# Attention, a cos-gated layer and a routed expert layer in one kernel: the loads of queries, keys and values reshaped, and the order of several steps changed

## The reference

```python
for c in range(nc):                                  # chunks of 32 queries
    k_full = concat([mem_k, k[l_start:r_end]]); v_full = concat([mem_v, v[l_start:r_end]])
    a = softmax(scale * q_c @ k_full.T)
    out[c] = a @ v_full
x = out as [3072, 512]
h = x @ w_in                                         # 512 -> 2048
x = (h * cos(h)) @ w_out                             # 2048 -> 512
compute = x @ w_skip > 0
e = argmax(x @ w_gate); g = max(softmax(x @ w_gate))
out = x; out[compute] += g * (relu(x @ w1[e]) @ w2[e])   # 512 -> 1024 -> 512
```

## Time and profile before

| | us |
|---|---|
| median of 3 runs | 840.38 (839.9 to 841.39) |
| the profiled execution's own time | 839.99 |
| its span | 838.4 |
| PE busy | 818.1 (98% of the span) |
| DVE busy, ACT busy | 508.7, 466.4 |
| bytes moved by DMA | 93.87 MB, mean 112 GB/s |

### The profile page before, as it was taken

One profiled execution on the slowest core, in us unless ns is written; L12 is line 12 of the kernel. 1 busy time (PEld: TensorE's weight loads), 2 busy tenths in 40 slices (PEclk: granted clock), 3 DMA queues, 4 the chain that ended last, 5 costly groups with the idle time before them and its releaser, 6 DMA issues.

```text
span 838.4 us, 19569 instructions
## 1 busy us (share of the span) xinstructions
PE 818.1 (98%) x8178; PEld 727.1 (87%) x8178; DVE 508.7 (61%) x1021; ACT 466.4 (56%) x824; POOL 75.7 (9%) x96
## 2 busy tenths in 40 slices
PE   5999999999999999999999999999999999999997
PEld 4888888888888888888888898889898988999996
DVE  3588755565565556555655655564644878855663
ACT  2588765566565557555655555565545656444441
POOL 0200000010001001000100010001121332211000
PEclk9999999999999999999999999999999999999999
DMA  7761032103220421221031103202004699566300
GB/s 290 267 209 65 27 113 65 64 27 114 69 65 22 140 68 61 83 96 64 26 114 65 64 26 139 65 2 76 2 13 175 219 382 367 198 229 249 120 15 27
DMA packets 42864, 93.87 MB, mean 112 GB/s; under 512 B 9487, under 2 KB 9487, under 8 KB 42768
## 3 DMA queue, kind: packets, MB, share of 16 engines
q1 hardware_dynamic: 39280, 86.23, 28.9%
q0 software_dynamic: 3488, 6.30, 2.2%
HBM read 78.16 MB, written 17.00 MB: 113 GB/s over the span
## 4 chain that ended last, share of the span: by engine, by line
PE 90%; DMA 4%; DVE 3%; issue 1%; ACT 1%; SPq 1%; POOL 0%; POOLq 0%; DVEq 0%
PE h_ps L891 31%; PE y_ps L905 31%; PE h_ps L1051 8%; PE y_ps L1065 8%; PE s_ps L773 2%; PE s_ps L810 2%; DMA raw_a<-w 2%; PE turn L833 1%; PE turn L823 1%; PE turn L788 1%; DMA k_pre<-qk 1%; PE s_ps L845 1%; DMA lists<-pairs,place 1%; PE turn L932 0%; PE y_ps L810 0%
## 5 line engine op out<-in xcount | busy, mean ns | idle before, releaser
L891 PE MATMUL h_ps<-xT_hi,in_hi 128*128 128x384 f32 x512 | 178.4, 348 | 0.0
L891 PE MATMUL h_ps<-xT_hi,in_lo 128*128 128x384 f32 x512 | 172.4, 337 | 0.0
L891 PE MATMUL h_ps<-xT_lo,in_hi 128*128 128x384 f32 x512 | 171.7, 335 | 0.0
L905 PE MATMUL y_ps<-out_hi,g_hi 128*128 128x512 f32 x384 | 150.9, 393 | 0.9 <-DVE g_lo L1448 0.7
L905 PE MATMUL y_ps<-out_hi,g_lo 128*128 128x512 f32 x384 | 151.6, 395 | 0.0
L905 PE MATMUL y_ps<-out_lo,g_hi 128*128 128x512 f32 x384 | 151.3, 394 | 0.0
L1145 ACT ACTIVATE hs<-h_ps 128x384 f32<-128x384 f32 x128 | 62.3, 487 | 154.0 <-PE h_ps L891 153.7
L1442 DVE TENSOR_SCALAR whole<-us 128x384 f32<-128x384 f32 x128 | 46.0, 359 | 132.2 <-ACT us L1146 130.4
L1169 ACT ACTIVATE us<-us 128x384 f32<-128x384 f32 x128 | 67.3, 525 | 68.4 <-DVE us L1444 68.0
L891 PEld LDWEIGHTS h_ps<-xT_hi,in_hi 128*128 128x128 f32 x512 | 96.4, 188 | 3.2
L891 PEld LDWEIGHTS h_ps<-xT_lo,in_hi 128*128 128x128 f32 x512 | 96.5, 188 | 2.3
(11 more groups left out here) (209 smaller groups left out, 1285.4 us busy)
## 6 DMA issues: line engine op xcount, KB each, us to landing
raw_a<-w SPq DMA_DIRECT2D x32, 512.0 KB, 7.6
raw_b<-w SPq DMA_DIRECT2D x32, 512.0 KB, 7.6
k_sb<-qk SPq DMA_DIRECT2D x22, 512.0 KB, 4.5
v_sb<-v SPq DMA_DIRECT2D x22, 512.0 KB, 3.7
x_mid<-x SPq DMA_DIRECT2D x24, 256.0 KB, 4.4
out<-x SPq DMA_DIRECT2D x24, 256.0 KB, 5.0
q_sb<-qk SPq DMA_DIRECT2D x22, 256.0 KB, 3.0
in_raw<-w_in SPq DMA_DIRECT2D x4, 1024.0 KB, 6.2
```

What stands on the lines that cost most here:

```text
L891: last = pe.matmul(h_ps[:, f % 2, 0:BN], w[:, dc, f * P:(f + 1) * P], x[:, half, dc, :], start=(n == 0), stop=(n == 3 * DC - 1))
L905: last = pe.matmul(y_ps[:, j, :], g[:, f % RING, j * P:(j + 1) * P], w[:, f, :], start=(f == 0 and n == 0), stop=(f == FT - 1 and n == 2))
```

## The change

1. **Loads.** Queries and keys of a tile come in one load into `qk_sb` [128, 3, 512] (6 KB for each partition), values in one load as before, 4 KB for each partition; views give the old shapes.
2. **Prologue.** The three orders are changed; the values of tile 1 go to `s_ps`; 64 instead of 32 small matmuls at the start; the first idle matmuls stand after x of tile 1; the first `w_in` split on ACT stands ahead of x of tile 0; the first load of `w_out` waits for the values of tile 1.
3. **Middle layer.** ACT makes `us` ahead of `hs`, with a semaphore `us_done` of its own, for which DVE's `fraction` waits; in the last f-step of block 7 `g_high` and `g_low` of the f-step before come first.
4. **Raw `w2` of slot 1** is loaded during block 7.
5. **Routing and slot 0.** Half of the turning of the gathered rows goes ahead of `ranks`; 4 idle matmuls are gone; the fourth `w1_low` of slot 0 stands after the first `eg_lo`.
6. **A slot with at most 128 rows** ends with one small matmul that raises `ey_full`, in place of a wait.

```diff
-PROLOGUE_PE = [("scores", 0), ("scores", 1), ("probs", 0), ("scores", 2), ("probs", 1), ("values", 0), ("values", 1),
-               ("probs", 2), ("x", 0), ("values", 2), ("x", 1), ("x", 2)]
-PROLOGUE_ACT = [("exp", 0), ("probs", 0), ("exp", 1), ("probs", 1), ("exp", 2), ("probs", 2), ("x", 0), ("x", 1),
-                ("w_in", 0), ("x", 2), ("w_in", 1), ("w_in", 2)]
-PROLOGUE_DVE = [("scores", 0), ("scores", 1), ("sum", 0), ("scores", 2), ("values", 0), ("sum", 1), ("values", 1),
-                ("sum", 2), ("values", 2), ("x", 0), ("x", 1), ("x", 2)]
+PROLOGUE_PE = [("scores", 0), ("scores", 1), ("probs", 0), ("scores", 2), ("probs", 1), ("values", 0), ("probs", 2),
+               ("values", 1), ("x", 0), ("values", 2), ("x", 1), ("x", 2)]
+PROLOGUE_ACT = [("exp", 0), ("probs", 0), ("exp", 1), ("probs", 1), ("exp", 2), ("probs", 2), ("w_in", 0), ("x", 0), ("w_in", 1),
+                ("x", 1), ("x", 2), ("w_in", 2)]
+PROLOGUE_DVE = [("scores", 0), ("scores", 1), ("sum", 0), ("scores", 2), ("sum", 1), ("values", 0), ("sum", 2),
+                ("values", 1), ("x", 0), ("values", 2), ("x", 1), ("x", 2)]
...
-        def values_bank(B):
-            return y_ps[:, 1:3, 0:HP * HD] if is_first(B) else s_ps[:, :, 0:HP * HD]
+        def values_bank(B, j):
+            return y_ps[:, 1:3, 0:HP * HD] if is_first(B) and j != 1 else s_ps[:, :, 0:HP * HD]
...
-            def load_qk(tile, to_q, to_k, ld):
-                sp.dma_start(to_q, qk[bass.ds(tile, 1), :, 0:HP * P].rearrange("a p n -> (a p) n")).then_inc(ld, 16)
-                sp.dma_start(to_k, qk[bass.ds(tile, 1), :, HP * P:].rearrange("a p n -> (a p) n")).then_inc(ld, 16)
+            def load_qk(tile, to, ld):
+                sp.dma_start(to.rearrange("p r n -> p (r n)"), qk[tile, :, :]).then_inc(ld, 16)
...
             load_in(0)
+            sp.wait_ge(v_full, 2)
             load_out(0)
             sp.wait_ge(v_full, 3)
...
+                    sp.wait_ge(t_full, use(B - 1, "x", BT - 1) + 1)
+                    carry(sp)
+                    load_raw2(1, 1, lambda w: w[1, :, :])
...
-                wait(sp, w2lo_done, 4 * (s - 1))
                 if isinstance(s, int) and s == 1:
 
                     load_lists()
                     sp.wait_ge(xg_ld[1], rows_landed(1))
-                for n in range(4):
-                    sp.dma_start(raw2[par][:, 2 * n:2 * n + 2, :],
...
+                else:
+                    wait(sp, w2lo_done, 4 * (s - 1))
+                    load_raw2(s, par, expert)
...
-                        wait(pe, v_free, j)
+                        wait(pe, s_free, (0, 3, 3)[j])
+                        wait(pe, v_free, (0, 0, 1)[j])
...
-            for n in range(32):
+            for n in range(64):
...
-                if (step, j) == ("values", BT - 1):
+                if (step, j) == ("x", 1):
                     keep_running(turn[:, 0, 0:P], 3)
...
-            keep_running(y_ps[:, 1, 0:P], 4)
...
+            pe.wait_ge(xg_ld[0], 32)
+            gathered_rows(0)
             pe.wait_ge(route_step, ROUTE * (BLOCKS - 1) + CHOSEN)
             ranks().then_inc(last_ranks_full, 1)
...
+            gathered_rows(1)
...
-                    pe.wait_ge(ey_full, 2 * s + 1)
-                    pe.sem_inc(ey_full, 1)
+                    pe.matmul(y_ps[0:32, 1, 0:NL], ident[:, 0:32], ident[:, 0:NL], start=True, stop=True).then_inc(ey_full, 1)
...
-                act.activation(hs[:, f % 2, :], h_ps[:, f % 2, 0:BN], ACT.Copy)
                 act.activation(us[:, f % 2, :], h_ps[:, f % 2, 0:BN], ACT.Copy, scale=1.0 / TWO_PI,
-                               bias=0.25).then_inc(h_free, 1)
+                               bias=0.25).then_inc(us_done, 1)
+                act.activation(hs[:, f % 2, :], h_ps[:, f % 2, 0:BN], ACT.Copy).then_inc(h_free, 1)
...
-                    chain_first = f == 1 and not has_router(B)
+                    chain_first = (f == 1 and not has_router(B)) or (f == FT - 1 and is_last(B))
...
             w1_low(0, 0, 2)
-            w1_low(0, 0, 3)
...
+                    if isinstance(s, int) and s == 0 and g == 0:
+                        w1_low(0, 0, 3)
                     w2_low(s, par, g)
```

More of the change, by code:

```diff
@@ L406, in tile_of, with queries_of, keys_of, values_of @@
             return BT * (B + 1) + j
[L408 to L412, removed]
+        def queries_of(t):
+            return t[:, 0, :].rearrange("p (h q) -> p h q", q=P)
+        def keys_of(t):
+            return t[:, 1:3, :].rearrange("p r (h c w) -> p (r h) c w", c=CPT, w=WIN)
+        def values_of(t):
+            return t.rearrange("p r (c n) -> p (r c) n", n=HP * HD)
         def par_of(half, j):
@@ L469, in _, with load_v @@
         def _(sp):
[L470 to L475 removed]
+            def load_qk(tile, to, ld):
+                sp.dma_start(to.rearrange("p r n -> p (r n)"), qk[tile, :, :]).then_inc(ld, 16)
+            def load_v(tile, to, ld):
+                sp.dma_start(to.rearrange("p r n -> p (r n)"), v[tile, :, :]).then_inc(ld, 16)
             def load_in(n):
@@ L552, in run, with load_raw2 @@
                     load_list(0, list_ld[0])
+            def load_raw2(s, par, expert):
+                for n in range(4):
+                    sp.dma_start(raw2[par][:, 2 * n:2 * n + 2, :],
+                                 expert(w2)[2 * n * P:(2 * n + 2) * P, :].rearrange("(c p) d -> p c d", p=P)
+                                 ).then_inc(raw2_ld[par][n], 16)
             for B in range(BLOCKS):
@@ L766, in attend @@
                     to = scores_banks(B, j)
-                    queries = q_pre[:, j - 1, :, :] if ahead else q_sb[:, :, :]
-                    windows = k_pre[:, j - 1, :, :, :] if ahead else k_sb[:, :, :, :]
+                    given = qk_pre[:, j - 1, :, :] if ahead else qk_sb[:, :, :]
+                    queries, windows = queries_of(given), keys_of(given)
                     for hp in range(HP):
@@ L803, in attend @@
                     carry(pe)
-                    to = values_bank(B)
-                    windows = v_pre[:, j - 1, :, :] if ahead else v_sb[:, :, :]
+                    to = values_bank(B, j)
+                    windows = values_of(v_pre[:, j - 1, :, :] if ahead else v_sb[:, :, :])
                     for hp in range(HP):
@@ L963, in _, with gathered_rows @@
             last_logits(2)
-            keep_running(y_ps[:, 1, 0:P], 4)
+            def gathered_rows(i):
+                for dc in (2 * i, 2 * i + 1):
+                    for a in range(2):
+                        c = (dc % 2) * SLOT + a * P
+                        pe.matmul(s_ps[:, i, c:c + P], xg[0][:, a, dc * P:(dc + 1) * P], ident[:, :],
+                                  start=(dc % 2 == 0 and a == 0), stop=False)
+            pe.wait_ge(xg_ld[0], 32)
+            gathered_rows(0)
             pe.wait_ge(route_step, ROUTE * (BLOCKS - 1) + CHOSEN)
             ranks().then_inc(last_ranks_full, 1)
-            pe.wait_ge(xg_ld[0], 32)
-            for dc in range(DC):
-                for a in range(2):
-                    c = (dc % 2) * SLOT + a * P
-                    pe.matmul(s_ps[:, dc // 2, c:c + P], xg[0][:, a, dc * P:(dc + 1) * P], ident[:, :],
-                              start=(dc % 2 == 0 and a == 0), stop=False)
+            gathered_rows(1)
             def last_rows(part, i, j, ends):
@@ L1191, in run @@
                         g_high(B, f - 1)
-                    elif has_router(B):
+                    elif f == 0 and has_router(B):
                         g_high(B - 1, FT - 1)
```

43 lines of the change are left out of this document (20 added, 23 removed).

## The result

The changed kernel takes 834.74 us (median of 5 runs, 831.13 to 835.18), the kernel before 840.38 beside it (838.19 to 841.39). The ratio is 0.9927, 95% interval [0.9906, 0.9948]: 5.6 us faster, where 8.6 were forecast. 834.74 lies inside the range of 828.0 to 836.0. The profiled execution took 834.37 us, its span is 832.7.

A forecast was written before the change was run, and what follows sets the result against it. PE was taken as the bound from 60 to 640 us. Gains of 5.2, 0.5, 0.7 and 2.15 sum to 8.6 us, from the profiled 839.99 to 831.4, or 831.8 against the median; range 828.0 to 836.0.

The forecast's parts named there:

- half a prologue: Rival: a longer PE stop or DVE setting the pace leaves a prologue gain of 2.5 us, 835.2 us; chance 0.17.
- no late gain: Rival: late stage gives nothing, as PE's wait for expert 1's rows and DMAs behind shift too; 834.6 us; chance 0.09.
- The stop: Prologue: PE's standstill without releaser, 1.38 us at 16.22 before, hits another place and costs 0 to 1.4, taken as 0.8.
- One of my own signs of being wrong: Ahead of L1006: prediction wrong if PE's wait there, forecast at about 1.2 us, passes the 2 us gained ahead of it.
- Prologue: Up to block 0: new orders, separate banks and less idle work start block 0 at 24.3; gain 5.2 us, ends 3.3 and 7.5.
- loads sooner: Rival, prologue: third keys land 1.5 us sooner, 1.0 counted as gained; 830.8 us; chance 0.08.
- Block 0 and middle layer: `us` first shortens the chain to `g_lo`; 0.5 us back in block 0, bounds 0 and 0.6, nothing in blocks 1 to 7.
- The `g_lo` wait of block 7: Last block: step 14's chain first removes the wait at 641.07, listed as 0.33, counted as 0.5 us.
- Last block to expert 1's rows: PE gets there 2.0 us sooner but rows only 0.5; gain 0.7, bounds 0.2 and 1.2, with a new 1.2 us wait.
- Slots 0 and 1: Small matmul removes a 0.45 us wait, early raw `w2` removes 1.7 ahead of slot 2; together 2.15, bounds 1.4 and 2.5.
- The clock: Prologue: PE, busy from 14.6, may reach 2.4 GHz around 20 us; rival with early, lasting rise: 829.5 us, chance 0.13.
- Slower: Rival, prologue: first `w_in` split holds up x of tile 0 if its load lands after 17.4; 843.4 at 29; chance 0.02.

The follow-up runs named there:

- after: The changed kernel itself, against the kernel before: 834.74 us, ratio 0.9927.
- the six: The six kernels that share the changed kernel's prologue code, itself included; their block 0 starts at 25.82, 25.01, 24.75, 24.74, 25.02 and 24.82 us.
- the last run: Changed kernel without small matmuls at the start, `w_in`'s first load held until three scores are done, expert 1's rows turned at the seventh product: 830.49 us, 0.9888.

## Why the prediction was right, and where its steps were off

The sign, the range and most places were right; the sum was 2.8 us too large in the account, in three terms. The case that I held for the likeliest, 831.8, was not what came: 834.74 is nearer to the sums of two rivals, half a prologue (its own 2.5 gives 834.5, not the 835.2 that stands there) and no late gain (834.6), and something of both mechanisms was there. The stop grew, and PE's new wait took back what was gained ahead of it. One of my own signs of being wrong came with it: that wait passes the 2 us.

- **Prologue, 5.2 forecast, 3.57 measured** (in this profile; 4.4 to 4.65 in the five others with the same prologue). The step that failed is the stop: "I take 0.8", at one place, with 1.4 as the end of its range. There are two, with 1.69 + 2.24 = 3.9. That the cause is a late block of instructions, put as an "if", is what the counts and packets showed. The 3.1 more of stops cost less than their length. The third keys landed at 10.91 us, as I had them (11.0), so the first stop, over at 9.98, lay mostly in a time in which PE had to wait for them anyway: the third scores start at 11.75 instead of 11.16, 0.6 later. And the clock was up at the end: the last twelve idle matmuls take from 24.24 to 25.82, 1.58 us, where the sum has 2.56 and the step to 24.3 took only a part of that off. The rival "loads sooner" did not come in this kernel. The orders themselves are worth 2.45 us, the clock's share in it included. One reading was off without harm: the wait for `x_sb` at 26.09 comes not from the shared banks but from the single buffer `x_sb`; after covers it with the six idle matmuls and keeps the 0.30.
- **The 64 small matmuls** got no price of their own. They move the first place from the scores of tile 2 into those of tile 1; without any, block 0 starts 4.1 us sooner (3.0 to 4.1 against the six) and the kernel is 5.3 us faster by the medians, 4.5 by the ratios. That is the largest single effect of the study.
- **Block 0 and middle layer, 0.5 forecast, 0.70 measured.** The size and the place were right, the wait was not: the one that was to go, for `g_lo` at 46.29, is there with 0.31 (42.12). The `up` group ahead of it starts 13.72 us behind block 0's first matmul instead of 14.23, the one behind it 18.80 instead of 19.45: 0.51 of the gain comes ahead of the wait, from steps with no listed wait, and 0.14 around it.
- **The `g_lo` wait of block 7, 0.5 forecast, 0.58 measured**: right, the wait is gone.
- **Last block to expert 1's rows, 0.7 forecast, -0.04 measured.** PE came to the turning as forecast; the rows did not. `lists` and `listed` took 5.04 + 3.01 us where the kernel before has 4.73 + 1.85 ahead of its `xg_b`. I took the DMAs at their old durations, with a lower bound of 0.2. Their sum was 6.7 to 8.2 in the ten chains of new kernels in which they stand; what makes them slower stays open.
- **Slots 0 and 1, 2.15 forecast, 1.60 measured.** The stretch to slot 2 gives 1.47, near the forecast 1.7; 0.2 of it are the small matmul at its end, the rest is the early `w2`, and is shown. Ahead of slot 1 I counted the whole wait of 0.45, and the stretch gives 0.13: the step behind a half slot goes only from 0.69 (before) or 0.68 (the run with the wait) to 0.48, where it is 0.23 in a dense stretch.
- **The clock** was up at 22.2, in place of "around 20", and in other profiles not steadily (below). *Slower* did not come: the first `w_in` landed at 4.12 + 13.3 = 17.4, as before, and its split cost nothing.

## What to carry to other kernels

A wait without a releaser inside a run of equal instructions is a stop of its own kind: count the engine's instructions to it, compare the distance of two such places, and look for the instruction queue's packet in the DMA view. In a start-up phase that fills the DMA queues, every instruction issued early "to warm up" brings the engine sooner to the next block, and a load asked for before it is needed delays that block; a load that is held back can in turn stand ahead of the next block, as in the last run, so look where it will lie. A gain ahead of a gather is worth only what the gather itself moves; follow the chain of the data before adding up PE's waits.

## What the runs showed of the hardware

**The granted clock and what PE did before.** In the profile of after the first recorded rise to the upper level is at 22.2 us, and PE had been busy from 16.95 on without a pause. Ahead of it the column says 1.00, but the durations are those of 1.2 GHz: 64 values took 1.19 us at 21.00 and 0.86 in the run without small matmuls, whose clock was up from 12.9. In five of the runs, with the same or nearly the same prologue, it rose at 13.5 to 14.4, about where the second stop begins, and fell again behind it. The kernel with the later turning, by windows:

```profile
14.00:17.40 3.40, 1.05 (x51) 0.81 (x46) 1.16 (x5) 0.74 (x2) 0.00 (x0) 1.00 0.32 115
17.40:20.90 3.50, 3.50 (x136) 2.67 (x134) 2.20 (x6) 1.85 (x4) 1.27 (x1) 0.51 0.18 28
20.90:24.70 3.80, 3.47 (x50) 2.99 (x33) 2.63 (x5) 2.29 (x5) 1.41 (x2) 1.00 0.96 357
```

A stop can thus cost more than its length: PE, busy again without a pause, runs at 1.2 GHz for 3.4 us. It need not: with the clock up, the level fell behind the five stops of 1.49 to 2.46 us and not behind the one of 1.84 in the last run, nor behind those of 1.02 and 1.14. The same fall came behind the wait of 2.1 us for expert 1's rows in four of the eight profiles that have it, and in none of the five with a wait of 0.8 to 1.1. With `hs` first, by windows:

```profile
666.40:669.80 3.40, 3.40 (x13) 3.01 (x12) 1.61 (x3) 2.40 (x4) 2.59 (x3) 0.51 0.81 254
669.80:672.00 2.20, 1.80 (x9) 1.18 (x7) 2.13 (x2) 0.69 (x1) 0.41 (x1) 1.00 1.01 389
```

It costs 1.6 us there (5.5 from the turning to slot 1 instead of 3.9). Why it falls in some executions and not in others with the same wait, the runs do not settle; nor was it tried whether a few idle matmuls in that wait would prevent it.

**The price of a late block** is 1.3 to 1.6 us behind its packet's end, besides the packet's own 0.9 to 1.1 us and whatever stands ahead of it. The data seem to pay too: the third keys, asked for at 1.84 us in all new kernels with whole loads, land at 10.1 to 10.9 where the packet runs at about 7 us, ahead of them, and at 9.1 to 9.2 in the three runs (32 small matmuls, none, the last one) in which it comes behind them, at 9.7 or later. So part of what fewer small matmuls give may be this; no run tried it alone.
